# Attention output with tokens on the partitions: norm by VectorE, transposes back by TensorE

## What is computed

```python
kv  = einsum('bhsd,bhse->bhde', k, v)
out = einsum('bhsd,bhde->bhse', q, kv)
out = out / sqrt(mean(out*out, axis=-1) + 1e-6) * g_norm
x   = out.transpose(0, 2, 1, 3).reshape(2304, 512)
h = x @ w_in;  x = (h * sigmoid(1.702*h)) @ w_out       # expert 1
h = x @ w_in2; x = softplus(h) @ w_out2                 # expert 2
```

## Time and profile before

| | |
|---|---|
| median of 3 runs | 858.57 us (858.33 to 858.64) |
| profiled execution | 856.86 us, span 855.0 us |
| TensorE (matmuls) busy | 840.9 us, 98% |
| VectorE, ScalarE, GpSimd busy | 434.0, 267.7, 203.7 us |
| DMA | 36.04 MB, most of it in the first 50 us |

### The profile page before, as it was taken

One profiled execution on the slowest core, in us unless ns is written; L12 is line 12 of the kernel. 1 busy time (PEld: TensorE's weight loads), 2 busy tenths in 40 slices (PEclk: granted clock), 3 DMA queues, 4 the chain that ended last, 5 costly groups with the idle time before them and its releaser, 6 DMA issues.

```text
span 855.0 us, 11290 instructions
## 1 busy us (share of the span) xinstructions
PE 840.9 (98%) x4064; PEld 708.6 (83%) x4064; DVE 434.0 (51%) x770; ACT 267.7 (31%) x493; POOL 203.7 (24%) x173
## 2 busy tenths in 40 slices
PE   7989999999999999999999999999999999999997
PEld 6877888998888888888888888888888888888896
DVE  2688434335333533354446755655565446555564
ACT  4664210211110211123334533433343333433343
POOL 2569420000000000004443532132222221222121
PEclk9999999999999999999999999999999999999999
DMA  9935310000000000002220200100010001000100
GB/s 295 335 140 190 120 54 1 2 2 1 0 1 1 0 0 0 0 0 74 99 74 0 74 1 1 49 0 0 0 49 0 0 0 49 0 0 0 49 2 25
DMA packets 13485, 36.04 MB, mean 42 GB/s; under 512 B 1680, under 2 KB 3216, under 8 KB 13456
## 3 DMA queue, kind: packets, MB, share of 16 engines
q1 hardware_dynamic: 12880, 35.39, 12.3%
q10 hardware_dynamic: 576, 0.27, 0.1%
HBM read 30.94 MB, written 4.72 MB: 42 GB/s over the span
## 4 chain that ended last, share of the span: by engine, by line
PE 95%; DVE 2%; issue 1%; DMA 1%; POOL 1%; ACT 0%; SPq 0%; POOLq 0%; DVEq 0%
PE ps L422 45%; PE ps L384 45%; PE ps L311 2%; PE ps L322 2%; DMA kv_in_sb<-k_v 1%; PE ps L336 1%; DVE hid L603 0%; DVE xy L617 0%; POOL sq_s L260 0%; POOL w_own L268 0%; PE ps L348 0%; DVE gs L686 0%; DVE xs L631 0%; PE ps L403 0%; DVE sq_s L625 0%
## 5 line engine op out<-in xcount | busy, mean ns | idle before, releaser
L686 DVE CAST gs<-hid 128x512 fp32r<-128x512 f32 (+1 forms) x160 | 83.0, 519 | 280.4 <-PE ps L422 279.0
L384 PE MATMUL ps<-xs,w_shared 128*128 128x512 f32 (+1 forms) x960 | 210.1, 368 | 0.0
L384 PE MATMUL ps<-xs,w_own 128*128 128x512 f32 (+1 forms) x960 | 206.4, 368 | 0.3 <-DVE xy L617 0.2
L384 PEld LDWEIGHTS ps<-xs,w_shared 128*128 128x128 f32 x960 | 168.8, 188 | 30.6
L384 PEld LDWEIGHTS ps<-xs,w_own 128*128 128x128 f32 x960 | 167.8, 188 | 31.3 <-DVE xs L633 0.8
L285 POOL TENSOR_TENSOR stage<-stage 128x512 f32<-128x512 f32 (+1 forms) x80 | 94.5, 1182 | 291.8 <-DVE stage L670 291.8
L539 ACT ACTIVATE hid<-ps 128x512 f32<-128x512 f32 (+1 forms) x80 | 44.5, 556 | 267.2 <-PE ps L384 261.9
L268 POOL TENSOR_TENSOR w_own<-stage,w_own 128x512 fp32r<-128x512 f32 x32 | 42.0, 1339 | 293.1 <-ACT w_own L473 293.0
L688 DVE TENSOR_TENSOR gs<-hid,gs 128x512 fp32r<-128x512 f32 (+1 forms) x160 | 106.1, 663 | 5.5
L422 PE MATMUL ps<-gs,w_own 128*128 128x512 f32 (+1 forms) x480 | 105.2, 368 | 0.2 <-DVE gs L686 0.2
L543 ACT ACTIVATE stage<-ps 128x512 f32<-128x512 f32 (+1 forms) x80 | 44.5, 556 | 194.1 <-PE ps L384 175.8
(11 more groups left out here) (45 smaller groups left out, 436.4 us busy)
## 6 DMA issues: line engine op xcount, KB each, us to landing
stage<-moe_w SPq DMA_DIRECT2D x32, 512.0 KB, 3.3
kv_in_sb<-k_v SPq DMA_DIRECT2D x16, 512.0 KB, 7.5
q_sb<-q_t SPq DMA_DIRECT2D x16, 288.0 KB, 6.3
out<-xy SPq DMA_DIRECT2D x18, 256.0 KB, 2.2
tail_sb<-k_v SPq DMA_DIRECT2D x3, 256.0 KB, 8.5
tail_sb<-k_v ACTq DMA_DIRECT2D x1, 256.0 KB, 5.0
g_col<-g_norm ACTq DMA_DIRECT2D x2, 0.2 KB, 6.7
hb_raw<-head_bcast ACTq DMA_DIRECT2D x1, 8.0 KB, 5.5
```

The lines of the kernel that those rows point to most:

```text
L384: mm = nc.tensor.matmul(bank, w[:, W_IN, wp, cols], xs[:, xp, k, 0:width], start=(k == 0 and (wp, xp) == (HI, HI)), stop=(k == KT - 1 and ...
L686: nc.vector.tensor_copy(gs[:, HI, s, :width], g).then_inc(g_hi_made, 1)
```

## The change

The raw output is formed the other way round: 128 columns of queries are stationary and K^T V (128 columns) moves, so tokens lie on the partitions. The 64 tail tokens of two units share one tile: each pair's odd unit has five tiles of 128 columns, the even one four. For that the queries have 64 zero columns behind (even units) or before them (odd units), and the host rolls the odd units' queries so that their tails come first. ScalarE squares straight from PSUM (`square`), VectorE sums each head's 64 squares along the free axis (`sum_squares`, now on VectorE), ScalarE takes the root (`root`), VectorE the reciprocal and the product with a broadcast operand (`scale`), all once a unit. Two rounds later TensorE transposes back with an identity (`turn`), and ScalarE multiplies by `g_norm` on the way to `xy` (`gain`). The sum and spread products, the split of the squares and their buffers are gone. K^T V has one PSUM bank in place of two and four SBUF copies in place of two. `split_high` of the first three tiles stands behind round 15, `gain(14)` and `gain(15)`.

```diff
@@ constants
-KV_BANK, RAW_BANK, SUMSQ_BANK, BCAST_BANK = 0, 2, 4, 6
+KV_BANK, RAW_EVEN, RAW_ODD, TURN_EVEN, TURN_ODD = 0, 1, 2, 4, 5
+LAST_TURNS = (0, 1)
-    SUM_LAG = 2
-    BCAST_LAG = 7
+    TURN_LAG = 2
         def hid_bank(f):
-            return HID_BANK + (f + 1) % HID_BANKS
+            return HID_BANK + (f + 3) % HID_BANKS
@@ SyncE, load_unit
                 if u >= UNIT_SLOTS:
-                    sp.wait_ge(raw_done, u - UNIT_SLOTS + 1)
-                sp.dma_start(q_sb[:, b, :], q_t[u]).then_inc(q_in[b], 16)
+                    sp.wait_ge(raw_done, (u - UNIT_SLOTS) // 2 * 2 + 2)
+                if u == 0:
+                    sp.wait_ge(pads_made, 2)
+                first = PAD if u % 2 else 0
+                sp.dma_start(q_sb[:, b, first:first + S], q_t[u]).then_inc(q_in[b], 16)
@@ GpSimd
-            for u in range(UNITS):
-                split_squares_low(u)
-                if u > UNITS - W_EARLY:
-                    split_low(u - 1 - (UNITS - W_EARLY))
-            for g in range(W_EARLY - 1, G_LATE - 1):
+            for g in range(G_LATE - 1):
                 split_low(g)
@@ TensorE
             def raw_output(u):
...
-                if u >= 1:
-                    pe.wait_ge(raw_copied, u)
-                for h in range(2):
-                    mm = nc.tensor.matmul(ps[:, RAW_BANK + h, 0:HALF], kv_sb[:, b, :],
-                                          q_sb[:, slot, h * HALF:(h + 1) * HALF], start=True, stop=True)
+                if u >= 2:
+                    pe.wait_ge(scaled, u - 1)
+                main, _ = q_tokens(u, slot)
+                for t in range(MAIN):
+                    cols = slice(t * P, (t + 1) * P)
+                    mm = nc.tensor.matmul(out_rows[:, cols], main[:, cols], kv_sb[:, slot, :],
+                                          start=True, stop=True)
+                if u % 2:
+                    for v in (u - 1, u):
+                        _, tail = q_tokens(v, v % UNIT_SLOTS)
+                        mm = nc.tensor.matmul(out_rows[:, FULL_ROWS:FULL_ROWS + P], tail,
+                                              kv_sb[:, v % UNIT_SLOTS, :], start=(v != u), stop=(v == u))
                 mm.then_inc(raw_done, 1)
+            def turn(u):
+                x = x_tok[:, u % 2]
+                to = columns(turn_bank(u), width_of(u))
...
+                pe.wait_ge(scaled, u + 1)
+                if 2 <= u < UNITS - 2:
+                    pe.wait_ge(x_made, u - 1)
+                if u == UNITS - 2:
+                    pe.wait_ge(kv_copied, 2 * UNITS)
+                for t in range(width_of(u) // P):
+                    cols = slice(t * P, (t + 1) * P)
+                    mm = nc.tensor.transpose(to[:, cols], x[:, cols], eye_sb[:])
+                mm.then_inc(turned, 1)
@@ TensorE, chunk
+                    if first and f in (1, 2):
+                        turn(UNITS - 3 + f)
+                        pe.wait_ge(x_made, UNITS - 4 + f)
                     if first and f == 3:
-                        late_broadcasts([UNITS - 1])
+                        pe.wait_ge(x_made, UNITS)
@@ ScalarE
-            def copy_and_square(u):
...
+            def square(u):
                 act.wait_ge(raw_done, u + 1)
+                if u >= 2:
+                    act.wait_ge(summed, u - 1)
+                nc.scalar.activation(sq_sb[:, u % 2, 0:width_of(u)], raw(u), ACT.Square).then_inc(squared, 1)
+            def root(u):
+                sums = rms[:, u % 2, 0:width_of(u) // D]
+                act.wait_ge(summed, u + 1)
+                nc.scalar.activation(sums, sums, ACT.Sqrt, bias=eps_col[:, :], scale=1.0 / D).then_inc(rooted, 1)
+            def gain(u):
+                p, tok = u % PAIRS, u // PAIRS * S
+                act.wait_ge(turned, u + 1)
+                if u % 2:
+                    nc.scalar.activation(xy[:, p - 1:p + 1, tok + FULL_ROWS:tok + S],
+                                         columns(turn_bank(u), FULL_ROWS + P, FULL_ROWS).rearrange(
+                                             "p (a n) -> p a n", a=2), ACT.Copy, scale=g_col[:, 0:1])
+                nc.scalar.activation(xy[:, p, tok:tok + FULL_ROWS], columns(turn_bank(u), FULL_ROWS),
+                                     ACT.Copy, scale=g_col[:, 0:1]).then_inc(x_made, 1)
+            act.wait_ge(consts_in, 48)
+            for u in range(UNITS + TURN_LAG):
                 if u + 1 < UNITS:
                     copy_kv(u + 1)
                 if u < UNITS:
+                    square(u)
+                if u >= TURN_LAG:
+                    gain(u - TURN_LAG)
+                if u < UNITS:
+                    root(u)
+                if u >= UNITS - W_EARLY + 2:
+                    split_high(u - (UNITS - W_EARLY + 2))
@@ VectorE
+            def sum_squares(u):
+                n = width_of(u) // D
+                dve.wait_ge(squared, u + 1)
...
+                nc.vector.tensor_reduce(rms[:, u % 2, 0:n],
+                                        sq_sb[:, u % 2, 0:n * D].rearrange("p (a d) -> p a d", d=D),
+                                        axis=AXIS.X, op=ALU.add).then_inc(summed, 1)
             def scale(u):
...
+                dve.wait_ge(rooted, u + 1)
+                nc.vector.reciprocal(inv, inv).then_inc(inv_made, 1)
...
+                nc.vector.tensor_tensor(x_tok[:, u % 2, 0:n * D].rearrange("p (a d) -> p a d", d=D),
+                                        raw(u).rearrange("p (a d) -> p a d", d=D),
+                                        inv.unsqueeze(2).to_broadcast([P, n, D]), ALU.mult).then_inc(scaled, 1)
```

More of the change, by code:

```diff
@@ L13 @@
 ACT = mybir.ActivationFunctionType
+AXIS = mybir.AxisListType
 P = 128
@@ L26, with build @@
 HID_SLOTS = 2
-def build(nc, q_t, k_v, g_norm, moe_w, moe2_w, head_bcast, out):
+def build(nc, q_t, k_v, g_norm, moe_w, moe2_w, eye, out):
     UNITS, _, S = q_t.shape
@@ L38, in build @@
     TAIL = S - MAIN * P
-    HALF = S // 2
+    FULL_ROWS = MAIN * P
+    PAD = P - TAIL
     CHUNK = 512
@@ L149, in build, with width_of, columns, raw @@
         LATE_AT = {2 * i + 1: G_LATE - 1 + i for i in range(4)}
[L153 to L166, removed]
+        def width_of(u):
+            return FULL_ROWS + P if u % 2 else FULL_ROWS
+        def columns(first_bank, width, first=0):
+            return ps[:, first_bank:first_bank + 2].rearrange("p a n -> p (a n)")[:, first:width]
+        def raw(u, first=0):
+            return columns(RAW_ODD if u % 2 else RAW_EVEN, width_of(u), first)
+        def turn_bank(u):
+            if u >= UNITS - 2:
+                return LAST_TURNS[u % 2]
+            return TURN_ODD if u % 2 else TURN_EVEN
+        def q_tokens(u, slot):
+            main = slice(P, P + FULL_ROWS) if u % 2 else slice(0, FULL_ROWS)
+            tail = slice(0, P) if u % 2 else slice(FULL_ROWS, FULL_ROWS + P)
+            return q_sb[:, slot, main], q_sb[:, slot, tail]
         def hid_bank(f):
-            return HID_BANK + (f + 1) % HID_BANKS
+            return HID_BANK + (f + 3) % HID_BANKS
         def steps_before(ci):
@@ L315, in raw_output @@
             def raw_output(u):
-                b, slot = u % 2, u % UNIT_SLOTS
+                slot = u % UNIT_SLOTS
+                out_rows = raw(u)
+                if u == 0:
+                    pe.wait_ge(pads_made, 2)
                 pe.wait_ge(q_in[slot], 16 * (u // UNIT_SLOTS + 1))
                 pe.wait_ge(kv_copied, 2 * (u + 1))
-                if u >= 1:
-                    pe.wait_ge(raw_copied, u)
-                for h in range(2):
-                    mm = nc.tensor.matmul(ps[:, RAW_BANK + h, 0:HALF], kv_sb[:, b, :],
-                                          q_sb[:, slot, h * HALF:(h + 1) * HALF], start=True, stop=True)
+                if u >= 2:
+                    pe.wait_ge(scaled, u - 1)
@@ L342, in broadcast @@
[L342 to L351, removed]
+                    pe.wait_ge(consts_in, 48)
@@ L353, in _ @@
+                pe.wait_ge(scaled, u + 1)
[7 more added lines that the diff above has]
+                mm.then_inc(turned, 1)
             kv_product(0)
-            for u in range(UNITS + SUM_LAG - 1):
+            for u in range(UNITS):
@@ L355, in _ @@
                 if u + 1 < UNITS:
                     kv_product(u + 1)
[L357 to L364, removed]
-                    broadcast(v)
-            def late_broadcasts(units):
-                for u in units:
-                    before = last_in(late_bank(u), u)
-                    if before is not None:
-                        pe.wait_ge(x_made, before + 1)
-                    broadcast(u)
+                raw_output(u)
@@ L374, in up @@
+                if u >= TURN_LAG:
+                    turn(u - TURN_LAG)
             def up(f, n0, ci, width, phase, tiles=range(KT)):
@@ L513, in _ @@
             copy_kv(0)
-            for u in range(UNITS + SUM_LAG):
+            act.wait_ge(consts_in, 48)
+            for u in range(UNITS + TURN_LAG):
                 if u + 1 < UNITS:
```

(14 more changed lines are left out.)

174 lines of the change are left out of this document (42 added, 132 removed).

## The result

| | before | changed |
|---|---|---|
| median | 858.61 us (858.33 to 859.15, 4 runs) | 866.0 us (864.08 to 868.16, 4 runs) |
| profiled execution | 856.86 us, span 855.0 | 867.3 us, span 865.5 |
| TensorE busy | 840.9 us, 98% | 841.8 us, 97% |
| fifth hidden product, f = 4, starts | 76.04 us | 86.53 us |

The ratio of the two kernels' runs is 1.0093, 95% interval 1.0079 to 1.0106: the change costs 0.9%, 7.4 us, where I had forecast no difference and a range up to 862.2 us. In the profiled execution it costs 10.4 us, and up(4) starts 10.5 us later: the prediction's measure, the start of that product, holds, and the experts' steady part lost nothing. The changed kernel also spreads over 4 us where the one before spreads over 1.

A forecast was written before the change was run, and what follows sets the result against it. TensorE, through the fifth hidden product's start (76.04 us), was taken to decide the time: rounds gain 0.9 us, the hand-off loses 1.0, sum +0.1 to +0.2 us, start 76.2. Forecast 858.7 us, 8-in-10 range 856.4 to 862.2.

The forecast's parts named there:

- What bounds the kernel, and the measure: TensorE never pauses from 76.0 us on; each us the fifth hidden product (76.04 us) shifts is a us of the total.
- TensorE's rounds: Attention rounds on TensorE: two units take 5.63 us against 5.74, with transposes at 0.11 us each.
- The loads: K, V and query loads in the rounds: query loads waiting for odd units cost nothing; unit 15's product starts by 48.4 us.
- The wait for the memsets: First query load, SyncE's queue: waits for two memsets, about 0.5 us; taken as 0 on unit 1's first product.
- the price if the cover were gone: Query loads in SyncE's queue: without about 4 us of queued loads, each pair of units would pay up to 2 us.
- ScalarE and VectorE: Attention rounds, two units: ScalarE 4.0 us and VectorE 4.9 us, both below 5.3 us and hidden.
- rival 2: Rounds: VectorE sets the pace if its sums cost 1.1 and 1.4 us; 861.9 us, chance 0.09.
- rival 3: Rounds: transposes cost a full f32 product; fifth hidden product at 83.6 us, total 866.1 us, chance 0.06.
- The hand-off: From unit 15's raw product to the fifth hidden product: 23.9 us where it was 22.9.
- The ring: Hand-off: ScalarE's gain and split, GpSimd's split, TensorE's product and transposes wait on each other, three times; TensorE waits 2.5 to 3.2 us.
- Rival 1: Hand-off: TensorE's clock falls in its waits; one fall +2.7 us, 861.4; all three +8, 867; chance 0.15.
- My own sign of being wrong: Hand-off: the prediction would be wrong if blocks of 12 matmuls took more than 2.8 us.

The follow-up runs named there:

- six buffers: Changed kernel with six buffers for K, V and queries in place of four (UNIT_SLOTS): 863.94 us; with the first three weight splits moved early too, 852.0 us.
- The pair wait alone: Kernel before, with a unit's query load waiting for the raw output of its pair's odd unit: 859.76 us against 857.78, ratio 1.0033.
- the filled pauses: Changed kernel with 12 extra unused matmuls ahead of each of the first three hidden products: 862.89 us.
- early splits: Changed kernel with ScalarE's first three weight splits back behind the squares of units 13 to 15: 855.14 us against 857.78 before, ratio 0.997; repeated, 856.17 us.

## Why the prediction was wrong

**What bounds the kernel, and the measure.** Right. Up(4) moved by 10.5 us and the profiled execution by 10.4.

**TensorE's rounds.** Right in size: a transpose takes 0.44 us in four, 0.55 in five, 0.11 us each, as taken; raw output 0.89 and 1.33. Two units take 5.45 us where nothing waits (5.63 forecast, 5.74 before). In the changed kernel it didn't matter, as forecast. The Trainium skill's figure ("TensorE: Matmul & The Clock Gate", Terms: four times faster for FP32), if it is meant against an f32 product, isn't what this trace shows: half of an f32 product's 0.222 us, not a quarter.

**The loads: the first step that failed.** "It costs nothing, since about 4 us of loads stand in the queues then." I counted bytes in the queue against one rate. The chain shows 9.75 and 6.21 us of loads in it, the windows a share of 0.78 to 0.99 where I had said above 1 until 48 us; at 0.99 they moved only 284 GB/s. With six buffers, so more loads outstanding, the share was 1.04 or 1.05 from 10 to 40 us, and TensorE waited 0.5 us at most for loads from 12 us on. The term was 0.9 us of gain and measured as 4.4 us of loss in the profile, 2.4 us in the mildest. The pair wait alone explains 2.0 us in the kernel before; the buffers give back 3 us at raw(15) and 4 in the time. The wait for the memsets, which I took at 0, holds a load back by 0.47 us. The prediction named the price if the cover were gone, up to 2 us a pair, and then gave it no place among the rivals.

**ScalarE and VectorE.** Mis-sized and harmless. The sum took 0.68 and 0.82 us for 0.60 and 0.73, the root of 8 elements 0.30 for 0.18, the reciprocal 0.20 for 0.1, the gain 0.69 for 0.59 and 0.36 for 0.25. Both engines stayed below the rounds of the changed kernel; rival 2 didn't happen, nor rival 3.

**The hand-off: right in mechanism, wrong in what I compared it with.** The ring is there step by step, with the three waits of TensorE of 3.30, 2.67 and 2.93 us (2.5 to 3.2 were forecast). At full clock it would have taken 24.6 us, or 25.0 by the filled pauses, for 23.9. But I set it against the old hand-off and saw 1.0 us. The change had also taken away what made the old one long, late spreads and GpSimd's splits of squares; without the ring the new one takes 17.2 us, in each of the four profiles with early splits and the transposes left where the change has them.

**The clock: the second step.** Rival 1, with a chance of 0.15, came true: in both profiles of the changed kernel, and by mean clock (0.990 to 0.997, where the kernel before has 0.997 to 1.000) in nearly all of its executions. It cost 4.0 us in the first profile, between one fall and the three that the range left out. I had the condition, three pauses longer than any in the old trace, where TensorE's longest in the hand-off is 1.34 us, and took "each has full work before it" as cover. It isn't: up(0) ran at 0.64 right behind the rounds, and with the pauses filled the clock stayed at 1.00. The Trainium skill's rule on transposes (same page, Part 4) isn't settled here. The clock stays at 1.00 through rounds with nine transposes in two units, where no pause is long. With the transposes ahead of the products, TensorE did nothing but transposes for 3.8 us, with pauses of 0.38 and 1.51 us between, and the clock was down behind them, while a pause of 1.58 us between products left it at 1.00. That agrees with the rule, but no run tells it from chance.

**The sum.** 53.17 - 0.9 + 23.9 was forecast as 76.2; it was 53.17 + 4.4 + 29.0 = 86.5. Of the 10.3 us between, 5.3 are the loads', 4.4 the clock's (4.0 by the filled pauses), 0.7 to 1.1 the ring's own. In the medians it is less, 866.0 for 858.7, since the first profile is among the slower executions. My own sign of being wrong, a block of 12 over 2.8 us in the hand-off, came true with 4.34. How much of the loads' part is the pairing and how much the varying service stays open; no run separates them within the changed kernel.

## What to carry to other kernels

When work is moved in front of or behind a hand-off, follow each engine's queue for a ring: B's item waits for A's, which stands behind something that waits for B. Compare the new hand-off with what it could be, not only with what it was. Count a queue's cover in requests outstanding as well as in bytes, and price each pause of TensorE that is longer than any in the trace with the half clock behind it. Filling a pause with unused work is a cheap test.

## What the runs showed of the hardware

- TensorE's granted clock fell behind ten of twelve pauses of 2.7 to 3.3 us in four profiles with the ring, though blocks of hidden products kept TensorE busy between them: PEclk was 0.50 to 0.65 over the product behind or its first 4 us, and twice it stayed at 1.00 (up(1) in the first profile, 2.99 us, and up(2) with up(3) without the wait for the memsets, 5.72 us). It fell behind a pause of 2.38 us (0.70 in the window after) and, with transposes ahead of the products, behind one of 1.51 us (0.50 from 60 to 62 us). Behind pauses of 1.58 to 1.60 us that came after hidden products it stayed at 1.00, in four profiles. A pause's length alone doesn't tell. The clock stayed low with work coming in again: from 76 to 81 us of the first profile it was 0.50.
- From 20 to 30 us the DMA engines moved 284 GB/s (the changed kernel) and 313 GB/s (early splits) at a busy share of 0.99, and 314 to 354 GB/s at 1.05 in the four profiles with six buffers: a full share isn't one rate. The windows don't hold the same loads, and what sets the rate at a given share stays open.
- A root over 8 elements took 0.30 us and a reciprocal over 8 took 0.20 us; once a unit, these fixed costs are most of the norm's small steps.
